# k and v pooled as whole keys on even and odd partitions, and attention scores by head on two halves of the array's rows

## The reference

```python
# q, k, v: (batch 8, heads 8, seq 576, head_dim 64)
k_p = k.reshape(B, H, 72, 8, D).mean(axis=3)      # pooled by 8 along the sequence
v_p = v.reshape(B, H, 72, 8, D).mean(axis=3)
scores = scale * q @ k_p.transpose(0, 1, 3, 2)    # 576 x 72 per head
attn = exp(scores - scores.max(-1)); attn /= attn.sum(-1) + 1e-9
x = attn @ v_p                                    # -> (4608 tokens, 512)
# soft MoE: logits = x @ phi (32 slots), softmax over tokens and over slots,
# 8 experts of 512 -> 1024 -> 512 on 4 slots each
# then x @ w_in (512 x 1024), softmax gate, layer norm, @ w_out (1024 x 512)
```

## Time and profile before

| | |
|---|---|
| median of 3 runs | 504.57 us (502.06 to 506.37) |
| the profiled execution | 501.91 us |
| its span on the core | 499.9 us |
| attention stage | up to about 205 us |
| share of the span: PE, DVE, POOL, ACT | 92%, 68%, 54%, 49% |
| mean granted TensorE clock | 0.97 |

### The profile page before, as it was taken

One profiled execution on the slowest core, in us unless ns is written; L12 is line 12 of the kernel. 1 busy time (PEld: TensorE's weight loads), 2 busy tenths in 40 slices (PEclk: granted clock), 3 DMA queues, 4 the chain that ended last, 5 costly groups with the idle time before them and its releaser, 6 DMA issues.

```text
span 499.9 us, 10814 instructions
## 1 busy us (share of the span) xinstructions
PE 459.4 (92%) x3925; PEld 371.4 (74%) x3925; DVE 341.8 (68%) x582; ACT 245.3 (49%) x521; POOL 271.0 (54%) x358
## 2 busy tenths in 40 slices
PE   2788999999999998779996999999999999999996
PEld 2677788888887887436664788878888888888875
DVE  7765878687877968264633899777777777777411
ACT  2345465565657465211222876555555665565410
POOL 0385666867676722005471333666666666666550
PEclk9998899999999999859999899999999999999999
DMA  9959496969869635689980014666666666666651
GB/s 294 262 165 306 163 274 233 315 171 296 196 255 246 250 108 195 230 289 338 399 328 1 1 43 70 134 125 132 126 143 145 141 133 132 134 133 132 132 127 42
DMA packets 125041, 91.75 MB, mean 184 GB/s; under 512 B 104520, under 2 KB 104528, under 8 KB 122960
## 3 DMA queue, kind: packets, MB, share of 16 engines
q1 hardware_dynamic: 125008, 91.32, 66.5%
HBM read 66.13 MB, written 9.44 MB: 151 GB/s over the span
## 4 chain that ended last, share of the span: by engine, by line
PE 38%; SPq 33%; DVE 16%; issue 5%; ACT 4%; POOL 2%; DMA 2%; DVEq 0%; ACTq 0%
SPq L417 29%; PE banks L1062 6%; SPq L406 3%; PE banks L1165 3%; PE banks L1281 3%; DVE attn L779 3%; PE banks L1261 3%; PE banks L1050 3%; DVE smax L775 3%; PE banks L1098 2%; PE banks L1118 2%; PE banks L1071 2%; PE banks L1134 2%; DVE mdiag L832 2%; ACT kblk L559 2%
## 5 line engine op out<-in xcount | busy, mean ns | idle before, releaser
L1369 PE MATMUL banks<-wo_hi,uh 128*128 128x512 f32 x288 | 112.6, 391 | 0.5 <-POOL ul L530 0.5
L1370 PE MATMUL banks<-wo_lo,uh 128*128 128x512 f32 x288 | 112.1, 389 | 0.0
L1371 PE MATMUL banks<-wo_hi,ul 128*128 128x512 f32 x288 | 112.1, 389 | 0.0
L530 POOL TENSOR_TENSOR ul<-u_col,uh 128x1024 fp32r<-128x1024 f32 x30 | 72.2, 2406 | 32.0 <-ACT uh L559 31.9
L450 POOL TENSOR_TENSOR attn<-attn,srec 128x576 f32<-128x576 f32 (+1 forms) x40 | 45.9, 1146 | 79.6 <-DVE srec L793 79.6
L1369 PEld LDWEIGHTS banks<-wo_hi,uh 128*128 128x128 f32 x288 | 54.1, 188 | 12.0 <-issue 0.9
L1371 PEld LDWEIGHTS banks<-wo_hi,ul 128*128 128x128 f32 x288 | 54.1, 188 | 11.3
L1370 PEld LDWEIGHTS banks<-wo_lo,uh 128*128 128x128 f32 x288 | 54.1, 188 | 11.1
L726 ACT ACTIVATE sq<-u,usum 128x1024 f32<-128x1024 f32 x36 | 41.5, 1153 | 41.6 <-DVE u L983 41.5
L1062 PE MATMUL banks<-kblk,qT 128*128 128x144 f32 (+1 forms) x320 | 50.0, 302 | 5.8 <-DVE attn L779 2.3
L973 DVE TENSOR_REDUCE nmax<-banks 128x1 f32<-128x1024 f32 x36 | 43.5, 1217 | 17.3 <-PE banks L1346 17.1
(11 more groups left out here) (162 smaller groups left out, 803.5 us busy)
## 6 DMA issues: line engine op xcount, KB each, us to landing
wslot<-in_moe_w SPq DMA_DIRECT2D x15, 2048.0 KB, 9.6
u_col<-u_blk SPq DMA_DIRECT2D x240, 64.0 KB, 2.1
kraw<-in_k SPq DMA_DIRECT2D x8, 1152.0 KB, 7.2
vraw<-in_v SPq DMA_DIRECT2D x8, 1152.0 KB, 5.4
qb<-in_q SPq DMA_DIRECT2D x32, 256.0 KB, 6.9
out<-osb SPq DMA_DIRECT2D x32, 256.0 KB, 2.5
wnine<-in_moe_w SPq DMA_DIRECT2D x1, 2048.0 KB, 9.5
win<-in_moe_w_in SPq DMA_DIRECT2D x1, 2048.0 KB, 7.6
```

What stands on the lines that cost most here:

```text
L530: pool.tensor_tensor(ul[par][:, :, :].rearrange("p c (q t) -> p (c q) t", q=4), v, uh[par][:, :, :].bitcast(F32).rearrange("p c (q t) -> p ...
L1369: pe.matmul(ps[4 + par], uh[par][:, c, :], wo_hi[:, c, :], start=(c == 0), stop=False)
L1370: pe.matmul(ps[4 + par], uh[par][:, c, :], wo_lo[:, c, :], start=False, stop=False)
L1371: last = pe.matmul(ps[4 + par], ul[par][:, c, :], wo_hi[:, c, :], start=False, stop=(c == FC - 1))
```

## The change

k and v are read by 64 rows of 72 tokens, nine whole keys each: the first five go to an even partition, the last four to the odd one behind it, in two DMAs. The fifth place of an odd partition is set to zero once and stays zero. The folds work on five keys a partition (1280, 640 and 320 elements, the first two in place), and the raw buffer is free for the next load only after the last. `rows_T` becomes three plain transposes, and the copies out of them are six. `kblk` loses its zeros; scores are eight matmuls of 72 columns, each on 64 rows of the array, head 0 of each pair into one bank, head 1 into the other. The short tile is multiplied with all 128 query columns. The order of keys inside a head changes, for k and v alike. Some small buffers move.

```diff
-QUADS = S * H // P // 4
+KEYS = SP * H // (P // 2)
+EVEN = KEYS // 2 + 1
+ODD = KEYS // 2
...
-        kraw = bump("kraw", [P, QUADS, 4 * D])
-        vraw = bump("vraw", [P, QUADS, 4 * D])
-        kq = bump("kq", [P, QUADS, D])
-        vq = bump("vq", [P, QUADS, D])
-        kp = bump("kp", [P, QUADS - 1, D])
+        kraw = bump("kraw", [P, EVEN, POOL * D])
+        vraw = bump("vraw", [P, EVEN, POOL * D])
+        kp = bump("kp", [P, EVEN, D])
+        vp = bump("vp", [P, EVEN, D])
...
-        kblk = [bump(f"kblk{i}", [P, PAIRS, 2 * SP]) for i in range(2)]
+        kblk = [bump(f"kblk{i}", [P, PAIRS, SP]) for i in range(2)]
...
-        s_view = banks[:, 0:2, :].rearrange("p a (j w) -> p (a j) w", j=2)
+        s_view = banks[:, 0:2, 0:PAIRS * SP].rearrange("p h (j c) -> p h j c", c=SP)
...
-        k_rows = k.rearrange("b h s d -> b (h s d)").rearrange("b (p n) -> b p n", p=P)
+        k_rows = k.rearrange("b h s d -> b (h s d)").rearrange("b (p n) -> b p n", p=P // 2)
...
-            return attn[0:n, par, t, :].rearrange("p (j w) -> p j w", w=PAIR)[:, :, 1:].rearrange("p j (h c) -> p j h c", c=SP)
+            return attn[0:n, par, t, :].rearrange("p (j w) -> p j w", w=PAIR)[:, :, 1:].rearrange("p j (h c) -> p h j c", c=SP)
...
-        def fold(engine, name, raw, quads, pooled, b, level):
+        def fold(engine, name, raw, pooled, b, level):
+            w = 4 * D >> level
             if level == 0:
-                engine.wait_ge(sem(f"{name}_in"), b * 16 + 16)
-                engine.tensor_tensor(raw[:, :, 0:2 * D], raw[:, :, 0:2 * D], raw[:, :, 2 * D:4 * D], ALU.add).then_inc(sem(f"{name}_fold"), 1)
+                engine.wait_ge(sem(f"{name}_in"), b * 32 + 32)
+                engine.tensor_tensor(raw[:, :, 0:w], raw[:, :, 0:w], raw[:, :, w:2 * w], ALU.add).then_inc(sem(f"{name}_fold"), 1)
             if level == 1:
                 engine.wait_ge(sem(f"{name}_fold"), b * 2 + 1)
+                engine.tensor_tensor(raw[:, :, 0:w], raw[:, :, 0:w], raw[:, :, w:2 * w], ALU.add).then_inc(sem(f"{name}_fold"), 1)
+            if level == 2:
+                engine.wait_ge(sem(f"{name}_fold"), b * 2 + 2)
                 if not (isinstance(b, int) and b == 0):
                     engine.wait_ge(sem(f"{name}T_ps"), b)
-                engine.tensor_tensor(quads[:, :, :], raw[:, :, 0:D], raw[:, :, D:2 * D], ALU.add).then_inc(sem(f"{name}_fold"), 1)
-            if level == 2:
-                engine.wait_ge(sem(f"{name}_fold"), b * 2 + 2)
-                first, second = (quads[:, n:n + QUADS - 1, :].rearrange("p (i x) d -> p i x d", x=2) for n in range(2))
-                engine.tensor_tensor(pooled[:, :, :].rearrange("p (x i) d -> p i x d", x=2), first, second, ALU.add).then_inc(sem(f"{name}_pooled"), 1)
+                engine.tensor_tensor(pooled[:, :, :], raw[:, :, 0:w], raw[:, :, w:2 * w], ALU.add).then_inc(sem(f"{name}_pooled"), 1)
...
+            def load_rows(raw, rows, b, loaded):
+                e, o = EVEN * POOL * D, ODD * POOL * D
+                sp.dma_start(raw[1::2, 0:ODD, :].rearrange("p m n -> p (m n)"), row(rows, b)[:, e:e + o]).then_inc(loaded, 16)
+                if isinstance(b, int) and b == 0:
+                    sp.wait_ge(sem("raw_zero"), 2)
+                sp.dma_start(raw[0::2, :, :].rearrange("p m n -> p (m n)"), row(rows, b)[:, 0:e]).then_inc(loaded, 16)
+
             def load_k(b):
-                sp.dma_start(kraw[:, :, :].rearrange("p m n -> p (m n)"), row(k_rows, b)).then_inc(sem("k_in"), 16)
+                load_rows(kraw, k_rows, b, sem("k_in"))
...
-                sp.wait_ge(sem("v_fold"), 2 * b + 2)
+                sp.wait_ge(sem("v_pooled"), b + 1)
                 load_v(b + 1)
...
+            pool.memset(vraw[:, ODD, :], 0.0).then_inc(sem("raw_zero"), 1)
...
                 for hh in range(2):
-                    for a in range(2):
-                        n, c = 5 - a, 5 * POOL * a
-                        i = b_head[a * D:(a + 1) * D, 0:n * D].rearrange("p (g j h m) -> p h j g m", g=n, j=PAIRS, h=2)[:, hh]
-                        last = copy(out(hh)[:, :, c:c + n * POOL].rearrange("p j (g m) -> p j g m", g=n), i, scale)
+                    for g, a, n in ((0, 0, 2), (0, 1, 2), (2, 0, 1)):
+                        i = b_head[a * D:(a + 1) * D, g * P:(g + n) * P].rearrange("p (g j h m) -> p h j g m", g=n, j=PAIRS, h=2)[:, hh]
+                        o = out(hh)[:, :, 4 * POOL * a:4 * POOL * (a + 1)].rearrange("p j (g m) -> p j g m", g=2)
+                        if g == 2:
+                            i, o = i[:, :, 0, 0::2], out(hh)[:, :, 8 * POOL:SP]
+                        last = copy(o, i, scale)
...
+            dve.memset(kraw[:, ODD, :], 0.0).then_inc(sem("raw_zero"), 1)
             dve.memset(vpad[:, :, :], 0.0)
             for i in range(2):
-                dve.memset(kblk[i][:, :, :], 0.0)
...
                 for j in range(PAIRS):
-                    last = pe.matmul(s_view[0:n, j, 0:2 * SP], qT[bit(tile)][:, j, 0:n],
-                                     kblk[par][:, j, :], start=True, stop=True)
+                    for hh in range(2):
+                        rows = slice(hh * D, (hh + 1) * D)
+                        last = pe.matmul(s_view[:, hh, j, :], qT[bit(tile)][rows, j, :], kblk[par][rows, j, :], start=True, stop=True,
+                                         tile_position=(hh * D, 0))
...
-            def rows_T(name, quads, pooled):
-
-
-                for x in range(2):
-                    for g in range(2):
-                        pe.matmul(b_head[:, (2 * x + g) * D:(2 * x + g + 1) * D], pooled[:, 4 * x + 2 * g:4 * x + 2 * g + 2, :].rearrange("p a d -> p (a d)"),
-                                  ident[:, x::2], start=True, stop=True)
-                for x, m in enumerate((QUADS - 1, 0)):
-                    last = pe.matmul(b_head[0:D, 4 * D:5 * D], quads[:, m, :], ident[:, x::2], start=(x == 0), stop=(x == 1))
+            def rows_T(name, pooled):
+
+                for g in range(3):
+                    m = min(2, EVEN - 2 * g)
+                    last = pe.transpose(b_head[0:m * D, g * P:(g + 1) * P], pooled[:, 2 * g:2 * g + m, :].rearrange("p a d -> p (a d)"), ident[:, :])
                 last.then_inc(sem(f"{name}_ps"), 1)
```

More of the change, by code:

```diff
@@ L109, in build @@
         qb, ql = [bump("qb0", [P, 4, DM])], [bump("ql0", [P, DM])]
-        kraw = bump("kraw", [P, QUADS, 4 * D])
-        vraw = bump("vraw", [P, QUADS, 4 * D])
-        kq = bump("kq", [P, QUADS, D])
-        vq = bump("vq", [P, QUADS, D])
-        kp = bump("kp", [P, QUADS - 1, D])
+        kraw = bump("kraw", [P, EVEN, POOL * D])
+        vraw = bump("vraw", [P, EVEN, POOL * D])
+        kp = bump("kp", [P, EVEN, D])
+        vp = bump("vp", [P, EVEN, D])
+        lt = [bump(f"lt{i}", [P, P]) for i in range(2)]
+        datT = bump("datT", [SP, 2, P])
         assert place[0] >= p1 + 2 * HALF
@@ L131, in build @@
         v72 = [bump(f"v72_{i}", [SP, H, D]) for i in range(2)]
-        lt = [bump(f"lt{i}", [P, P]) for i in range(2)]
         smax = [bump(f"smax{i}", [P, H]) for i in range(2)]
@@ L331, in _ @@
         def _(sp):
+            def load_rows(raw, rows, b, loaded):
[4 more added lines that the diff above has]
+                sp.dma_start(raw[0::2, :, :].rearrange("p m n -> p (m n)"), row(rows, b)[:, 0:e]).then_inc(loaded, 16)
             def load_k(b):
-                sp.dma_start(kraw[:, :, :].rearrange("p m n -> p (m n)"), row(k_rows, b)).then_inc(sem("k_in"), 16)
+                load_rows(kraw, k_rows, b, sem("k_in"))
             def load_v(b):
-                sp.dma_start(vraw[:, :, :].rearrange("p m n -> p (m n)"), row(v_rows, b)).then_inc(sem("v_in"), 16)
+                load_rows(vraw, v_rows, b, sem("v_in"))
             def load_q(b, par, tiles=range(TILES)):
@@ L439, in k_fold @@
             def k_fold(b, level):
-                fold(pool, "k", kraw, kq, kp, b, level)
+                fold(pool, "k", kraw, kp, b, level)
             def v_fold(b, level):
-                fold(pool, "v", vraw, vq, vp, b, level)
+                fold(pool, "v", vraw, vp, b, level)
             def norm(tile):
@@ L449, in norm @@
                 pool.wait_ge(sem("srec"), num(tile) + 1)
-                pool.tensor_tensor(a, a, srec[bit(tile)][0:n, :].rearrange("p (j h) -> p j h", h=2)[:, :, :, None].to_broadcast([n, PAIRS, 2, SP]), ALU.mult) \
+                pool.tensor_tensor(a, a, srec[bit(tile)][0:n, :].rearrange("p (h j) -> p h j", h=2)[:, :, :, None].to_broadcast([n, 2, PAIRS, SP]), ALU.mult) \
                     .then_inc(sem("attn_ready"), 1)
@@ L762, in _ @@
             for level in range(3):
-                fold(dve, "k", kraw, kq, kp, 0, level)
+                fold(dve, "k", kraw, kp, 0, level)
             dve.wait_ge(sem("ident_ready"), 1)
@@ L769, in sub_max @@
                 n, par, g = ROWS[tile[2]], bit(tile), num(tile)
[L770 to L771 removed]
+                sc = s_view[0:n]
```

(5 more changed lines are left out.)

25 lines of the change are left out of this document (10 added, 15 removed).

## The result

| | before | changed |
|---|---|---|
| median | 503.56 us (4 runs, 502.06 to 506.37) | 531.37 us (4 runs, 529.35 to 538.63) |
| ratio | | 1.056, interval 1.049 to 1.063 |
| profiled execution | 501.91 us, span 499.9 | 538.63 us, span 536.5 |
| mean granted clock | 0.969 | 0.876 |

The profiled execution of the changed kernel is the slowest of its runs; the three others of the table and two further ones (532.27 and 535.80 us) have mean clocks of 0.888 to 0.914, so they differ from before in the same way, a little less.

A forecast was written before the change was run, and what follows sets the result against it. TensorE was taken as the bound, with DVE the next wall. Six batches at 1.5 us (9.0), batch 1 (1.2), batch 0 (0.8 and 0.5) and the last scores (0.3) gave about 12 us, so 492.5 us, range 484 to 508.

The forecast's parts named there:

- What bounds: Attention stage's middle batches: TensorE is the bound, 112.32 of 114.28 us in flight, with DVE next at 82%.
- Transposes of k and v: TensorE: three transposing records take 0.56 us for 1.41, saving 0.85 us twice per batch, 1.7 us.
- Scores on halves: Scores groups on TensorE: the halves load and multiply side by side, 0.93 us a group against 1.08.
- B: Rival, every scores group: the halves' loads run one after the other, +2.5 us per batch, about 522 us; chance 0.13.
- C: Rival, scores: pairs side by side, each half's load behind its own matmul; 505 to 509 us, milder 498 to 503; chance 0.13.
- Sum: -0.26 us per batch: Scores on TensorE: full tiles' change of shape, +0.13, and gain of 0.02 each, with the short tile's gain of 0.19.
- A clock under 1.00: Sign of being wrong: a granted clock under 1.00 in the attention stage's middle batches; no size or chance given.
- DVE's wall: DVE lets only about 0.5 us of k's saving and 1.0 of v's through: 1.5 of 1.96 us per batch.
- Folds and loads: POOL's folds stay level, 5.27 us against 5.30; loads issued some 0.8 us later stay hidden.
- Copies on ACT: Six copies for four, 1.54 us against 1.13, twice a batch; charged at 0.1 us per batch.
- Start: First batches: batch 0 gains 0.8 us from k and 0.5 from v, batch 1 gains 1.2.
- The sum: Whole kernel: 11.8, say 12 us saved, from 504.57 to 492.5 us; chance 0.64 for 487 to 498.

The follow-up runs named there:

- e9: The kernel before with only v's folds on POOL moved one step later: 495.50 us, ratio 0.988.
- e1: The changed kernel with the whole-array scores of before, so only k's and v's new transposes remain: 498.61 us against 500.83, ratio 0.994.
- e2: The kernel before with only the scores changed to eight matmuls on two halves of the rows: 516.31 us against 500.83.
- e3: The changed kernel with each half-row scores matmul streaming 144 columns in place of 72: 503.44 us against 500.83, ratio 1.003.
- e5: The changed kernel with k's and v's three transposes done as plain matmuls against the identity, six records for three: 524.93 us against 501.04.
- e6: The changed kernel with each of k's and v's three transposes done twice over the same place: 526.18 us against 501.04.
- e8: New transposes, whole-array scores, k's copies one step earlier, and v's folds one step later: 489.01 us against 501.62, ratio 0.975.
- e7: The changed kernel with the four scores matmuls of the lower half ahead of the upper half's four: 529.66 us against 501.04, ratio 1.058.

## Why the prediction was wrong, point by point

1. *What bounds.* TensorE, by 112 of 114 us in flight: right as a reading, wrong as a conclusion. e9 takes no work from TensorE and gains 0.7 us a batch. The earlier trace rows had it: the 2.4 us for lt, passed over as "hardly waits", are four waits of 0.6 us, one in each batch, and they hang on DVE's dense stretch. Being in flight is not being paced.
2. *Transposes of k and v.* 0.56 us forecast for a group, 0.48 measured in e1 (97.38 to 97.86) and 0.38 for v; 1.9 us a batch off TensorE. Right, and a little better.
3. *Scores on halves.* The unknown cost came out near the end I took: pairs side by side, 1.05 us from start to start where 0.93 was forecast; with the change of shape ahead of it the gain is nil, as e2's batches show, and B and C did not happen. The step that failed is another: "Sum: -0.26 us per batch". It priced the records at a granted clock of 1.00 that it took over from the earlier trace rows as if the clock were given. By its own working the group's streaming halves (8 pairs of 72 columns in place of 8 of 144) while its length nearly stays, because loads set the pace; and the clock fell, to 0.73 from 1.00 between 60 and 200 us. With the columns doubled again (e3) it is 0.95. A clock under 1.00 stood among the signs of being wrong, and not among the rivals. It should have been the slower rival: at the lower level a group of transposes takes 1.33 us against 0.77, and the seven batches of this stage took a fifth longer (180.7 us against 148.8).
4. *DVE's wall.* The place was right, the price was off: 0.65 us a batch felt in e1, not 1.5. I had let v's whole saving through. DVE's stretch "without a gap" has the slot maximum at 0.93 us and mdiag at 1.25 us in it, taken as work; in e9 they take 0.16 and 0.22 us, so 1.8 us of them were spent beside POOL's folds (1.5 us between e1 and e8), and with that gone the batch is 21.3 us, near the 21.4 that the forecast named. That this number comes out is luck: it takes a move that the change does not have.
5. *Folds and loads.* 2.90, 1.54 and 0.86 us against 2.92, 1.55 and 0.79 forecast; between 50 and 200 us no engine waited for k's or v's load. Copies on ACT: 1.51 us for six (forecast 1.54). Right.
6. *Start.* With the transposes alone the first slot maximum comes at 55.12 us against 57.90: 2.8 us, forecast 2.5. Right.
7. *The sum.* e1 is what the prediction described, less the halves: its profiled execution is 7 us shorter than that of before, its median 0.6%. Forecast 12. The change as it is: plus 28. The halves alone cost 9 to 20 us, the transposes alone gain 2, both together cost 28. That they meet in the clock is seen (from 60 to 200 us 0.94 in e2, 1.00 in e1, 0.73 together); why the new transposes, harmless alone, add so much to the halves stays open after e5 and e6.

The Trainium skill's advice on row tiling (TensorEngine Tiling (Array Packing), Overview) is a speed-up of up to two for a contraction of 64 rows. The trace agrees that two halves run side by side, with records 7 ns apart. It does not agree on the speed-up: 1.11 us against 1.15, since a pair of halves still needs 0.11 us for its fp32 weight loads of 128 columns, where a whole-array record of 144 columns needs 0.12. The warning that the prediction left unused is in the Trainium skill's TensorE: Matmul & The Clock Gate, The HAM clock gate: the clock depends on how busy the engine has been of late. Here the engine was in flight for 24.00 of 24.00 us at a granted clock of 0.51, so "busy" must not be read as the PE row of a profile. Part 4 of that page of the Trainium skill says that transposes do not bring the full clock; in e1, where transposes took the place of plain matmuls, the granted clock in the middle batches is 1.00, and on the halves the profiled executions of e5 and e6 (0.90 and 0.75) go the page's way. And for the two small DVE operations the Trainium skill's page SBUF — State Buffer (SBUF: two separate sides) has the rule, an exclusive lock on the ports that DVE and POOL share, held for a whole instruction, where the DVE operation has two SBUF inputs or is in a two-port mode; e1's end times, within 0.03 us of POOL's, agree.

## What to carry to other kernels

Price an edit to TensorE twice: by its length, and by what the stage would take at the lower level of the clock, if the edit leaves the engine fewer columns in nearly the same time. In a group that is paced by its weight loads, columns are cheap: 144 in place of 72 took 1.25 us in place of 1.11 a group here, and brought the kernel from 531 to 503 us. Look at where the records of the clock begin before kernels are compared by its mean. And where a small DVE operation shows 1 us in one place and 0.2 in another, look at what POOL was doing: moving v's folds by one step was worth 6 us here, with the whole-array scores of before.

## What was not expected of the hardware

- Two matmuls on the upper and lower 64 rows, fp32, 128 stationary columns: loads and matmuls start 7 ns apart by their single records, from pair to pair 0.11 us. On the same half one behind the other they need 0.11 us each, and with four matmuls on one half ahead of four on the other, the second half joins in with the fifth of the first's eight records (1.62 us for a group).
- The granted clock fell to 0.5 for stretches of 7 to 24 us while matmul records followed one another without a gap (76 to 100 us: PE busy 24.00 of 24.00), and came back by itself. From 60 to 200 us it had a mean of 0.73, and 0.95 with twice the columns in the same records.
- A DVE operation of 0.16 to 0.22 us lasts as long as the POOL operation that runs beside it: 1.05 and 0.84 us in e1, 0.16 and 0.22 in e8.
- Ahead of its first record (between 16 and 54 us in these kernels) the clock is shown as 1.00, while groups take their length of the lower level: 2.91 us at 27.09 us in e7, where the upper level has 1.62.
